# Attention of two batches ahead of the first channel stage, the second channel weight split inside it, and token mixing without an attention output

## The reference

```python
def _attn_ref(q, k, v):                       # q, k, v: [4, 8, 576, 64]
    q_s = softmax(q, over the 64 of a head); k_s = softmax(k, over the 576 rows)
    kv = np.einsum('bhsd,bhse->bhde', k_s, v)
    return np.einsum('bhsd,bhde->bhse', q_s, kv)
def _moe_ref(x, w_tok1, w_tok2, w_ch1, w_ch2):  # x: [4, 576, 512], 8 heads side by side
    h = np.maximum(x.transpose(0, 2, 1) @ w_tok1, 0.0) @ w_tok2     # 576 -> 256 -> 576
    u = x + h.transpose(0, 2, 1)
    return u + np.maximum(u @ w_ch1, 0.0) @ w_ch2                   # 512 -> 1536 -> 512
```

## Time and profile before

| | |
|---|---|
| 3 runs | 834.49, 836.6, 837.54 us; median 836.6 |
| profiled execution: span, first to last instruction | 824.8 us |
| own total time of the profiled execution | not given beside the span; the median of the runs is 11.8 us above the span |
| PE busy / weight load | 767.7 us (93%) / 688.7 us (84%) |
| DVE, ACT, POOL busy | 339.3, 223.1, 128.6 us (41%, 27%, 16%) |
| mean granted clock of PE | 0.979 |

### The profile page before, as it was taken

The page is one execution under the profiler, slowest core; times in us unless marked ns, Lnnn a source line. Parts: engine busy times, 40 slices in busy tenths (PEclk is TensorE's granted clock), DMA queues, the critical chain, the costliest instruction groups (busy, mean ns, idle before and its releaser), DMA issues.

```text
span 824.8 us, 15898 instructions
## 1 busy us (share of the span) xinstructions
PE 767.7 (93%) x4941; PEld 688.7 (84%) x4942; DVE 339.3 (41%) x620; ACT 223.1 (27%) x384; POOL 128.6 (16%) x155
## 2 busy tenths in 40 slices
PE   3789999999999999999999996688999999999994
PEld 3658999999999999899999996666888888888883
DVE  5687542436432436522342223825534422362221
ACT  2642123103123013222021132024524422352221
POOL 4201120002020002010000041321212211211211
PEclk9899999999999999999999998699999999999998
DMA  8680404001405002200015001066332501111000
GB/s 172 226 224 2 87 1 116 1 1 30 86 0 114 0 20 49 47 10 19 0 31 204 21 11 35 1 239 226 140 129 93 194 27 51 35 35 51 33 13 8
DMA packets 67868, 57.32 MB, mean 69 GB/s; under 512 B 51485, under 2 KB 53149, under 8 KB 67841
## 3 DMA queue, kind: packets, MB, share of 16 engines
q1 hardware_dynamic: 64320, 47.52, 20.4%
q0 software_dynamic: 3520, 9.44, 3.5%
HBM read 48.73 MB, written 10.31 MB: 72 GB/s over the span
## 4 chain that ended last, share of the span: by engine, by line
PE 83%; DVE 9%; DMA 3%; issue 2%; ACT 2%; SPq 1%; DVEq 0%; ACTq 0%; POOL 0%; POOLq 0%
PE bank L517 33%; PE bank L654 14%; PE bank L631 14%; PE bank L483 4%; PE bank L498 3%; PE bank L435 3%; DVE kmax L885 2%; PE bank L642 2%; PE bank L527 2%; PE bank L461 2%; DMA kb<-in_k_dram 1%; PE bank L472 1%; PE bank L538 1%; PE bank L618 1%; DVE wc_l L1025 1%
## 5 line engine op out<-in xcount | busy, mean ns | idle before, releaser
L517 PE MATMUL bank<-u_h,wc_h 128*128 128x288 f32 x384 | 120.8, 315 | 0.6 <-DVE hid_l L991 0.6
L517 PE MATMUL bank<-hid_h,wc_h 128*128 128x288 f32 x384 | 116.4, 303 | 0.0
L517 PE MATMUL bank<-hid_l,wc_h 128*128 128x288 f32 x384 | 113.2, 295 | 0.0
L517 PE MATMUL bank<-u_h,wc_l 128*128 128x288 f32 x384 | 113.1, 294 | 0.0
L517 PE MATMUL bank<-u_l,wc_h 128*128 128x288 f32 x384 | 113.0, 294 | 0.0
L517 PE MATMUL bank<-hid_h,wc_l 128*128 128x288 f32 x384 | 112.9, 294 | 0.0
L754 ACT ACTIVATE hid_h<-bank 128x288 fp32r<-128x288 f32 x96 | 39.2, 410 | 230.3 <-PE bank L517 230.3
L991 DVE SCALAR_TENSOR_TENSOR hid_l<-bank,hid_h 128x288 fp32r<-128x288 f32 x96 | 43.3, 454 | 129.7 <-ACT hid_h L754 129.6
L517 PEld LDWEIGHTS bank<-u_h,wc_h 128*128 128x128 f32 x384 | 72.1, 188 | 2.7 <-DVE hid_l L991 1.5
L631 PE MATMUL bank<-w1s_h,xgT_h 128*128 (+1 forms) x172 | 71.2, 414 | 2.9 <-DVE xgT_l L1206 1.5
L517 PEld LDWEIGHTS bank<-u_l,wc_h 128*128 128x128 f32 x384 | 72.2, 188 | 0.9
(11 more groups left out here) (196 smaller groups left out, 1234.8 us busy)
## 6 DMA issues: line engine op xcount, KB each, us to landing
w1raw<-in_moe_w_dram SPq DMA_DIRECT2D x20, 512.0 KB, 4.5
w2raw<-in_moe_w_dram SPq DMA_DIRECT2D x20, 512.0 KB, 5.3
w_stage<-in_moe_w_ch_dram SPq DMA_DIRECT2D x8, 768.0 KB, 6.6
vb<-in_v_dram SPq DMA_DIRECT2D x32, 144.0 KB, 3.6
x_rows<-x1n SPq DMA_DIRECT2D x24, 192.0 KB, 2.1
kb<-in_k_dram SPq DMA_DIRECT2D x24, 144.0 KB, 3.5
qb<-in_q_dram SPq DMA_DIRECT2D x24, 144.0 KB, 3.4
kraw<-in_k_dram SPq DMA_DIRECT2D x2, 576.0 KB, 6.3
```

The lines of the kernel that those rows point to most:

```text
L517: last = pe.matmul(to, lhsT, rhs, start=(m == 0), stop=(m == len(mms) - 1))
```

## The change

The head now holds the attention of batches 0 and 1 (groups 0 to 3), with keys, queries and values of all four groups loaded at the start; the values of groups 0 and 1 are loaded by ACT's queue, all others by SP's. In turn the loop of batch 0 holds no attention, only the `u` tiles of batch 1. The token mixing is reassociated: `mixed` multiplies the queries by the first token weight and `h1` multiplies that by `kvd`, so `xT` and `xs` are gone, and each `u` tile adds the product of `kvd` and `qT` by a third matmul. ACT writes `u[0]` and DVE `u[1]` straight from PSUM. The first channel weight is split in the head (high by ACT, low by DVE for slabs 0 and 2, by POOL for 1 and 3). The second is split in the `hid` chunks of batch 0: high by ACT after chunks 3, 5, 8 and 10, low by POOL, through two staging buffers; `y` chunks start when all four low slabs are there. The table `AT` is shifted.

```diff
+                kraw = [sb(raw, f"kraw{b}", [PS, NG, HG, NI, DH]) for b in range(2)]
+                qraw = [sb(raw, f"qraw{b}", [PS, NG, HG, NI, DH]) for b in range(2)]
...
-            xT = sb(part1, "xT", [P, KD, S])
+            with ExitStack() as second_stage:
+                w2_stage = [sb(second_stage, f"w2_stage{x}", [P, CH]) for x in range(2)]
             kb = sb(part1, "kb", [PS, NI, DG])
-            vb = sb(part1, "vb", [PS, HG, NI, DH + 1])
             qb = sb(part1, "qb", [PS, NI, DG])
-            qT = sb(part1, "qT", [P, CG, S])
-            xs = sb(part1, "xs", [PS, NI, DG])
+            vb = [sb(part1, f"vb_{x}", [PS, HG, NI, DH + 1]) for x in "eo"]
+            qT = sb(part1, "qT", [P, NG, CG, S])
+            mix = sb(part1, "mix", [P, CG, TOK])
...
-            ("qrec2", 0): 7, ("kv", 0): 9, ("qT01", 0): 11, ("qT23", 0): 12, ("xT01", 0): 13, ("xT23", 0): 13,
-            ("xs01", 0): 14, ("xs2", 0): 14, ("h1", 0): 15,
-            ("kmax", 1): 11, ("kmax2", 1): 11, ("mT", 1): 12, ("ksub", 1): 13, ("ksub2", 1): 13, ("kexp", 1): 13,
-            ("kexp2", 1): 13, ("qmax", 1): 14, ("qmax2", 1): 14, ("qexp", 1): 14, ("qexp2", 1): 14, ("qrec", 1): 14,
-            ("qrec2", 1): 15, ("kv", 1): 15, ("qT01", 1): 17, ("qT23", 1): 18, ("xT01", 1): 19, ("xT23", 1): 20,
-            ("xs01", 1): 21, ("xs2", 1): 22, ("h1", 1): 23,
+            ("qrec2", 0): 7, ("kv", 0): 9, ("qT01", 0): 10, ("qT23", 0): 11, ("mix", 0): 12, ("h1", 0): 13,
+            ("kmax", 1): 12, ("kmax2", 1): 12, ("mT", 1): 13, ("ksub", 1): 14, ("ksub2", 1): 14, ("kexp", 1): 14,
+            ("kexp2", 1): 14, ("qmax", 1): 14, ("qmax2", 1): 15, ("qexp", 1): 15, ("qexp2", 1): 15, ("qrec", 1): 16,
+            ("qrec2", 1): 16, ("kv", 1): 16, ("qT01", 1): 18, ("qT23", 1): 19, ("mix", 1): 20, ("h1", 1): 22,
...
+            for n in range(2 * NG):
+                load_raw(kraw[n // NG], k, n % NG, n // NG, k_first[n])
+                load_raw(qraw[n // NG], q, n % NG, n // NG, q_first[n])
+                if n == 0:
+                    sp.dma_start(wt1[:, :, :], w_tok1.rearrange("(p i) t -> p i t", p=PS)).then_inc(tok_w_in, 16)
+            sp.dma_start(wt2_raw, w_tok2.rearrange("(m p) s -> p m s", p=P)).then_inc(wt2_in, 16)
+            for j in range(KD):
+                sp.dma_start(w_stage[:, j, :], w_ch1[j * P:(j + 1) * P, :]).then_inc(stage_in[j], 16)
             sp.wait_ge(kv_ready, 1)
+            load_values(vb[0], 1, 0, v_first[2])
+            for x, j in enumerate(W2_ORDER):
+                if x == 0:
+                    sp.wait_ge(mix_ready, 1)
+                elif x == 1:
+                    sp.wait_ge(kv_ready, 2)
+                    load_values(vb[1], 1, 1, v_first[3])
                 else:
+                    sp.wait_ge(wc2_lo, x - 1)
+                sp.dma_start(w2_stage[x % 2][:, :].rearrange("p (c n) -> p c n", c=3),
+                             w_ch2.rearrange("(c p) n -> p c n", p=P)[:, 3 * j:3 * j + 3, :]).then_inc(stage2_in[x % 2], 16)
+            sp.wait_ge(wc2_lo, 4)
+            load_kv(2, 0)
+            load_q(2, 0)
...
+            def mixed(n, g):
+                pe.wait_ge(qn_done, 2 * n + 2)
+                pe.wait_ge(tok_w_in, 16)
+                if not early(n):
                     pe.wait_ge(h1_done, n)
+                elif n >= NG:
+                    pe.wait_ge(h1_done, n - 1)
+                for c in range(CG):
+                    for i in range(NI):
+                        last = pe.matmul(mix_bank(n, g)[:, c * TOK:(c + 1) * TOK], queries(n)[:, i, c * P:(c + 1) * P], wt1[:, i, :],
+                                         start=(i == 0), stop=(i == NI - 1))
+                last.then_inc(mix_ready, 1)
+            def h1(n, g):
+                pe.wait_ge(mix_done, n + 1)
+                pe.wait_ge(kvd_done, n + 1)
                 for m in range(KT):
+                    for c in range(CG):
+                        last = pe.matmul(mix_bank(n, g)[:, m * DG + c * P:m * DG + (c + 1) * P], mix[:, c, m * P:(m + 1) * P], kvd[:, g, c, :],
+                                         start=True, stop=True)
                 last.then_inc(h1_ready, 1)
...
-            def u_tile(bn, j):
+            def u_tile(bn, j, first=False):
                 half, c = j // KD, j % KD
                 if j == 0:
                     pe.wait_ge(h1_done, NG * bn + NG)
+                    pe.wait_ge(qT_done, 4 * (NG * bn + NG))
                     pe.wait_ge(wt2_ready, 1)
-                if j < 2:
-                    pe.wait_ge(xs_done, 3 * NG * (bn + 1))
-                else:
+                if j >= 2:
                     pe.wait_ge(u_done, 2 * KD * bn + j - 1)
+                part = slice(half * HS, (half + 1) * HS)
                 for m in range(KT):
+                    pe.matmul(u_bank(first, j)[:, 0:HS], h1T[:, m, c * P:(c + 1) * P], wt2[:, m, part], start=(m == 0), stop=False)
+                pe.matmul(u_bank(first, j)[:, 0:HS], kvd[:, c // CG, c % CG, :], qT[:, c // CG, c % CG, part],
+                          start=False, stop=True).then_inc(u_ready, 1)
+            def chunk(b, idx, first=False):
                 half, kind, i = chunk_of(idx)
                 to = bank[idx % 2][:, 0:HS]
-                if kind == "hid" and i == 0:
+                if first and idx == 0:
+                    pe.wait_ge(u_done, 2 * KD)
+                    pe.wait_ge(wc1_lo, 2)
+                    pe.wait_ge(wc1_lo_pool, 2)
+                elif kind == "hid" and i == 0:
                     pe.wait_ge(u_done, 2 * KD * b + KD * (half + 1))
+                if first and idx == NC1:
+                    pe.wait_ge(wc2_lo, 4)
                 pe.wait_ge(chan_done, NCB * b + idx + 1)
...
+            steps(("mT", 0), ("ksub", 0), ("kv", 0), ("mT", 1), ("qT01", 0), ("qT23", 0), ("ksub", 1), ("mix", 0), ("kv", 1), ("h1", 0),
+                  ("mT", 2), ("qT01", 1), ("qT23", 1), ("ksub", 2), ("mix", 1), ("h1", 1))
             for j in range(2 * KD):
-                u_tile(0, j)
-            pe.wait_ge(ch_split, 8)
+                u_tile(0, j, first=True)
+            steps(("kv", 2), ("mT", 3), ("qT01", 2), ("qT23", 2), ("ksub", 3), ("mix", 2), ("kv", 3), ("h1", 2),
+                  ("qT01", 3), ("qT23", 3), ("mix", 3), ("h1", 3))
             for idx in range(HEAD):
-                chunk(0, idx)
-            with pe.Fori(0, LAST) as b:
-                batch(b, True)
-            batch(LAST, False)
+                chunk(0, idx, first=True)
+            pe.wait_ge(h1_done, 2 * NG)
+            batch(0, True, False, first=True)
+            with pe.Fori(1, LAST) as b:
+                batch(b, True, True)
+            batch(LAST, False, False)
...
+            def mix_out(n, g):
+                act.wait_ge(mix_ready, n + 1)
+                act.activation(mix[:, :, :], mix_bank(n, g)[:, :].rearrange("p (c t) -> p c t", c=CG), ACT.Copy).then_inc(mix_done, 1)
...
+            def u_out(b, bn, j, first=False):
+                half, c = j // KD, j % KD
+                if not first:
+                    act.wait_ge(chan_done, NCB * b + NCH * half + NC1 + c + 3)
+                act.wait_ge(u_ready, 2 * KD * bn + j + 1)
+                act.activation(u[0][:, c, half * HS:(half + 1) * HS], u_bank(first, j)[:, 0:HS], ACT.Copy).then_inc(u_hi, 1)
...
+                    if first and idx in (3, 5, 8, 10):
+                        split_second((3, 5, 8, 10).index(idx))
...
+            def load_values(dst, b, g, landed):
+                for h in range(HG):
+                    act.dma_start(dst[:, h, :, 0:DH], v[b, g * HG + h, :, :].rearrange("(p i) d -> p i d", p=PS)).then_inc(landed, 16)
+            def split_first(*js):
+                for j in js:
+                    act.wait_ge(stage_in[j], 16)
+                    act.activation(wc1[0][:, j, :], w_stage[:, j, :], ACT.Copy).then_inc(wc1_hi, 1)
+            def split_second(x):
+                j = W2_ORDER[x]
+                act.wait_ge(stage2_in[x % 2], 16 * (x // 2 + 1))
+                if j < 2:
+                    act.wait_ge(kv_ready, NG + j + 1)
+                else:
+                    act.wait_ge(ksub_done, 2 * (j + 1))
+                act.activation(wc2[0][:, 3 * j:3 * j + 3, :].rearrange("p c n -> p (c n)"), w2_stage[x % 2][:, :], ACT.Copy).then_inc(wc2_hi, 1)
...
+            load_values(vb[0], 0, 0, v_first[0])
+            load_values(vb[1], 0, 1, v_first[1])
             steps(0, "kexp", "kexp2", "qexp", "qexp2", "qT01", "qT23")
-            steps(1, "qexp", "qexp2", "kexp", "kexp2")
-            steps(0, "xs01", "xs2")
+            steps(1, "kexp", "kexp2", "qexp", "qexp2")
+            steps(0, "mix", "h1")
...
-            stage_hi(0, 1, 2)
-            steps(0, "h1")
             steps(1, "qT01", "qT23")
-            stage_hi(3)
-            steps(1, "xs01", "xs2")
-            stage_hi(4, 5, 6, 7)
-            steps(1, "h1")
+            steps(2, "kexp", "kexp2", "qexp", "qexp2")
+            steps(1, "mix", "h1")
```

(84 more changed lines are left out.)

318 lines of the change are left out of this document (135 added, 183 removed).

## The result

The changed kernel takes 848.7 us (844.61 to 851.28, 4 runs), the kernel before 837.07; the ratio is 1.0135 with an interval of 1.0081 to 1.0188: slower by 1.4%, at the upper end of my range (829 to 849) and on the side I had given 0.36. Its profiled execution took 851.28 us with a span of 849.6, so 1.7 us lie outside the span and not 11.8.

A forecast was written before the change was run, and what follows sets the result against it. PE was taken as the bound, busy nearly all the time in the batches but idle 21 us in the head. Span 824.8 + 5.8 (head, batch 0) - 3.4 (batches 1, 2) = 827.2, plus 11.8 outside it: 839.0 us, range 829 to 849.

The forecast's parts named there:

- the likeliest case: Whole kernel: 839.0 us, 0.3% slower, inside what measurement can tell from no change; forecast's chance 0.45, own range 834 to 845.
- my 827.2: Forecast span of the changed kernel in us: 824.8 + 5.8 (head and batch 0) - 3.4 (batches 1 and 2).
- the price of ACT's 8 issues: Head: ACT issues the values of groups 0 and 1, 4608 pieces of 256 bytes, in about 10 us.
- Rival (b): Head: values on ACT's queue land late, at 20 to 25 us, delaying kv0; 840.6 to 845.6 us; chance 0.23.
- the walk's 87.4: Head: stepping through the engines' lists in written order, the first chunk starts at 87.4 us, 65.0 before.
- the wait of the `y` stage for POOL and two buffers: Batch 0: first `y` chunk waits for POOL's low slabs, starting 25.4 us after the first chunk; 6.4 us lost.
- -1.7 forecast: Batches 1 and 2: 117.6 us each against 119.3 before, 3.4 us won in the two.
- The small term in it: Batches 1 and 2: group 1's key maxima run after chunk 12 instead of 11, removing PE's 0.7 us wait.
- The 11.8 us outside the span: Whole kernel: the median of the runs lies 11.8 us above the profiled span, carried over to the forecast time.
- Rival (a): Head packs tighter: first chunk starts near 80, 7.4 us less, 831.6 us, faster; chance 0.22.
- Rival (c): Head and `y` wait: PE's clock falls to 1.2 GHz more often, 4 to 6 us in all, 844 us; chance 0.10.

The follow-up runs named there:

- the one with all mends and no jump: Changed kernel with values on SP, low slabs on DVE, slab 3's high copy behind group 3's query transposes, PE's loop written out: 824.96 us, ratio 0.9846.
- the two edits of ACT's order: Slab 3's high copy behind group 3's transposes, on values-on-SP kernel: 832.91 us; second token weight's copies behind group 1's, on split-slabs kernel: 818.49 us.
- the second profile: The kernel before, unchanged, run and profiled again: 838.38 us, ratio 0.9993, span 837.7 us.
- the fastest kernel: Mended, loop-free kernel with two second-weight slabs split at the head's end, plus ACT's second-token-weight copies behind group 1's query transposes: 818.49 us, ratio 0.9775.

## Why the prediction came out as it did

The direction and the range held, the likeliest case did not: I had 0.3% slower and "no change", it is 1.4%. That the time lies inside the range is luck. No case of mine held an engine blocked by its issues, and what kept the time under 849 is a gain that I had at nothing, the jump below: by the 17.6 us that the change costs without jumps it would have stood at 837.1 + 17.6 = 854.7. The span is 22.4 us above my 827.2, and that splits by my own steps like this.

- *The head.* 12.7 us of the error. The step that failed is the price of ACT's 8 issues, "about 10 us by that row": I took a rate from SP's four issues, where little was outstanding, and kept them off the path. They took 21 us, and what counts is that ACT computes nothing meanwhile. Rival (b) looked at the right place with the wrong mechanism: it made the transfer late. The run with group 0 alone on ACT has that mechanism pure, at 1.7 us; both together cost 13.1 by the run with the values on SP, so the blocked issue is 11.4, with the 1.3 us of the table load behind it. With the values on SP the walk's 87.4 was 88.2.
- *Batch 0.* 99.8 forecast, 100.3 measured; the wait of the `y` stage for POOL and two buffers came at 25.4 of 25.4 us, and the clock fell after it. Moving the low slabs to DVE gave back 5.3 us, so this term was really on the path.
- *The attention taken out of batch 0* is worth about what the trace said. Between the kernel before without jumps and the one with all mends and no jump, the head grows by 21.5 us (64.2 to 85.7) and batch 0 shrinks by 20.6 (115.7 to 95.2). PE's idle time in the old head bought nothing: it was 21.0 us there and is 20.2 in the new one. I put that down to the written order and to the attention's own chain through four engines; the two edits of ACT's order bear out the first, and nothing here tests the second.
- *Batches 1 and 2.* -1.7 forecast; 119.3 to 117.5 is -1.8. The small term in it was wrong: PE still waits 0.7 us for the key maxima, so the rest saved more than I gave it.
- *Batch 2* is 4.5 us above the forecast, the jump. That term was missing altogether, because the first profile of the kernel before had no such stop. In usual executions the kernel before pays two (5.8 + 5.6 us of batch time) and the changed one, whose batch 0 stands outside the loop, pays one (4.5). So a part of the change that I priced at nothing gave back about 7 us (12.7 - 5.5 by the times of the kernels with the loop written out).
- *The rest* is 4.7 us longer than 320.7 in this execution, in code that didn't change; over the 13 profiles of all these kernels it took 320.7 to 325.6. One small operation of DVE's routing took 6.97 us while POOL split expert weights, where the longest of the same group took 2.24 us before:

```profile
L1165 DVE TENSOR_TENSOR cc<-cc x5: 178/180/6971, 534.2 to 537.3; 128x18 f32<-128x18 f32 x5
```

PE's wait for it ran from 4.6 to 12.1 us over these profiles, but its next wait (for `oh`) moves against it: together they are 10.9 to 13.7, and 13.2 here against 11.2 in the first profile. That is 2.0 of the 4.7 us; PE's busy time is another 2.3 (292.4 against 290.1). I count it as chance, without a run that shows its cause.
- *The 11.8 us outside the span* were not there: 1.7 us are, and the other 10 are what usual executions are longer than the profiled one, by the second profile mostly the jumps. Forecasting 827.2 + 11.8 hid a missing term behind a false constant.

Rival (a), a first chunk near 80, was not met by any order tried: 83.7 in the fastest kernel. Rival (c) was half right: the clock cost 2.6 us at `mixed` of group 0 in some executions and not in others, and it fell after the `y` wait.

That the jump causes the stop is shown by the two kernels with only PE's loop written out; that PE fetches its code again there is what the traces suggest. The profile's instruction queue carries packets of 16 KB, 33 to 35 in the kernels with a loop on PE and 30 in those without. In the second profile of the kernel before, two of them lie in each of the two stops or at its start, and a third right behind it (stop 188.7 to 193.3 us, packets from 189 to 190 and from 193 to 194). The changed kernel's one stop, 326.0 to 328.9, has one at its start (326 to 327) and one right behind it (329 to 330). The quick first profile of the kernel before has none from 180 to 200 us and from 300 to 325, and only 17 in all, and it stopped nowhere; why that execution fetched so little stays open.

## What to carry to other kernels

An engine that computes should not issue transfers when many are outstanding: price an issue by what stands in the queue then, not by a row from a quiet place, and treat the engine as busy for it. When the profile's span lies far from the median of the runs, look for a second profile before trusting either; the gap here was worth more than the change. Moving work under an idle engine doesn't fill the idle time by itself: here 20.6 us moved cost 21.5. With its values on SP the change was level with the kernel before; a clear gain came only with the order of ACT's copies and the place of the splits, and it is 7.1 us when both kernels have PE's loop written out. A loop on the busiest engine is worth a run of its own: its two jumps cost 12.7 us in the kernel before, more than the change gained at its best.

## What the runs showed of the hardware

- An issue on ACT took 0.65 to 0.95 us for the first four value transfers (576 rows of 256 bytes each) and 3.6 to 5.0 for the next four, while SP issued 14 large ones. With four issues in all, ACT was through in 3.1 us. On SP four such issues took 4.8 us near the queue's start, 7.2 later in the same kernel, and 12.8 behind five large ones beside ACT's four. What limit holds an issue is not shown.
- Transfers of ACT's queue landed 14.0 us after issue (median) beside SP's, where the same four, third in SP's queue and issued from 1.99 us on, were there for a `kv` at 13.84.
- PE stood 2.8 to 4.6 us after a jump back of its loop, with nothing waited for, and ran at half the clock for some time after (granted 0.50), in every profile of a kernel with that loop but the first; written out, 12.7 us less in the kernel before and 5.5 in the changed one.
